# Dense bf16 matmuls in a recurrence on TensorE, one reordered step on VectorE, and two groups of loads issued later

## What is computed

```python
for t in range(S):                      # r, k, v: [B, H, S, D]; w, u: [H, D]
    cur = einsum('bhd,bhe->bhde', u[None] * kt, vt)
    y[:, :, t] = einsum('bhd,bhde->bhe', rt, state + cur)
    state = w[None, :, :, None] * state + einsum('bhd,bhe->bhde', kt, vt)

logits = x @ w_gate                     # x: [3072, 384]; each token to one of 8 experts,
h = maximum(x[mask] @ w1[e], 0.0)       # 384 tokens an expert, by falling logit
out[mask] = h @ w2[e]

h = maximum(maximum(x @ w1, x @ w2), x @ w3)
return h @ w_out                        # [3072, 384]
```

## Time and profile before

| | |
|---|---|
| Median of 3 runs | 818.34 us (815.5 to 818.6) |
| The profiled execution | 818.57 us, its span 816.5 us |
| TensorE busy, share of the span | 94% |
| VectorE | 57% |
| ScalarE | 28% |
| GpSimd | 20% |
| Moved by DMA | 68.64 MB, mean 84 GB/s |

### The profile page before, as it was taken

One profiled execution on the slowest core, in us unless ns is written; L12 is line 12 of the kernel. 1 busy time (PEld: TensorE's weight loads), 2 busy tenths in 40 slices (PEclk: granted clock), 3 DMA queues, 4 the chain that ended last, 5 costly groups with the idle time before them and its releaser, 6 DMA issues.

```text
span 816.5 us, 18498 instructions
## 1 busy us (share of the span) xinstructions
PE 771.2 (94%) x7502; PEld 738.2 (90%) x7502; DVE 461.5 (57%) x1083; ACT 230.9 (28%) x518; POOL 166.3 (20%) x203
## 2 busy tenths in 40 slices
PE   7999999999636999999999999999999999999996
PEld 6899999999526999999999999999999999999995
DVE  5554545452486778647666764766676477344231
ACT  5232332323402214203411521341152133134121
POOL 7644444450013002102101110210121011201001
PEclk9555555555558999999999999999999999999998
DMA  8996765200023022004103100500310040400000
GB/s 203 255 283 204 208 182 174 71 31 27 14 78 107 1 89 97 30 1 175 39 0 134 49 29 0 183 29 0 154 29 29 8 175 30 148 37 30 1 1 29
DMA packets 18198, 68.64 MB, mean 84 GB/s; under 512 B 3296, under 2 KB 7264, under 8 KB 16096
## 3 DMA queue, kind: packets, MB, share of 16 engines
q1 hardware_dynamic: 9312, 28.53, 12.9%
q0 software_dynamic: 5376, 34.61, 11.7%
q10 hardware_dynamic: 3456, 4.72, 1.6%
HBM read 58.41 MB, written 9.44 MB: 83 GB/s over the span
## 4 chain that ended last, share of the span: by engine, by line
PE 90%; DVE 4%; DMA 2%; ACT 1%; issue 1%; POOL 0%; POOLq 0%; SPq 0%
PE bank L1083 21%; PE bank L1085 20%; PE bank L1084 20%; PE bank L987 5%; PE bank L1000 5%; PE bank L1016 4%; PE bank L1050 3%; PE bank L967 3%; PE bank L950 3%; PE bank L1010 2%; DMA rkv<-in_rkv 2%; PE bank L1079 1%; DVE one_row L680 1%; ACT rk L489 1%; PE bank L930 1%
## 5 line engine op out<-in xcount | busy, mean ns | idle before, releaser
L1083 PE MATMUL bank<-xh,w1h 128*128 128x384 f32 x192 | 67.0, 349 | 0.0
L1083 PE MATMUL bank<-hh,w2h 128*128 128x384 f32 x192 | 66.9, 348 | 0.0
L401 POOL DMA_INDIRECT w1r<-in_w,w_row x8 | 8.5, 1064 | 283.0 <-PE bank L1085 231.5
L1085 PE MATMUL bank<-xh,w1l 128*128 128x384 f32 x192 | 64.5, 336 | 0.0
L1085 PE MATMUL bank<-hh,w2l 128*128 128x384 f32 x192 | 64.5, 336 | 0.0
L1084 PE MATMUL bank<-hl,w2h 128*128 128x384 f32 x192 | 64.3, 335 | 0.0
L1084 PE MATMUL bank<-xl,w1h 128*128 128x384 f32 x192 | 64.2, 335 | 0.0
L429 POOL DMA_INDIRECT out<-ot,idsc x24 | 23.8, 993 | 171.9 <-ACT ot L539 167.6
L862 DVE SCALAR_TENSOR_TENSOR hl<-bank,hh 128x384 fp32r<-128x384 f32 x64 | 35.3, 553 | 38.3 <-ACT hh L515 38.3
L515 ACT ACTIVATE hh<-bank 128x384 fp32r<-128x384 f32 x64 | 31.4, 491 | 83.2 <-PE bank L1085 82.1
L987 PE MATMUL bank<-middle,rk 48*64 48x48 f32 x384 | 51.3, 305 | 0.0
(11 more groups left out here) (182 smaller groups left out, 2056.0 us busy)
## 6 DMA issues: line engine op xcount, KB each, us to landing
rkv<-in_rkv SPq DMA_DIRECT2D x24, 576.0 KB, 7.1
rk<-in_rk SPq DMA_DIRECT2D x48, 192.0 KB, 4.6
x_rows<-ysb ACTq DMA_DIRECT2D x24, 192.0 KB, 4.0
m0r<-in_m SPq DMA_DIRECT2D x3, 384.0 KB, 17.3
m1r<-in_m SPq DMA_DIRECT2D x3, 384.0 KB, 9.0
m2r<-in_m SPq DMA_DIRECT2D x3, 384.0 KB, 6.1
mor<-in_m_out SPq DMA_DIRECT2D x3, 384.0 KB, 6.4
xg<-x_rows,idg POOLq DMA_INDIRECT x24
```

The costliest lines, as they stand in the source:

```text
L1083: pe.matmul(out, wh_, ah, start=first, stop=False)
L1085: return pe.matmul(out, wl_, ah, start=False, stop=last)
```

## The change

1. A table `DENSE` and a function `dense(times)`: matmuls of `ones16` (128x128, bf16) with `later16` taken four times (512 columns), into bank 0, whose result is overwritten by the scores. `scores(u)` issues them behind its two waits and ahead of its matmuls: 16 for units 2 and 9, two for every other unit from 1 on, none for unit 0.
2. On VectorE the scaling of unit 1 no longer stands ahead of the mask, first half and dot sums of unit 0, but behind them. All other units keep their order.
3. On SyncE `un` and `wg` are issued behind the loads of unit 1, no longer behind those of unit 0.
4. The twelve loads of the shared weights are issued behind the load of the last unit.

```diff
+DENSE = {2: 16, 9: 16}
@@ SyncE
                 load(u)
-                if u == 0:
+                if u == 1:
                     sp.dma_start(un[:].rearrange("p h d -> p (h d)"), u_d.partition_broadcast(P)).then_inc(s_const, 16)
                     sp.dma_start(wg[:], wg_d.rearrange("(k p) e -> p k e", p=P)).then_inc(s_const, 16)
@@
                 load(u)
-                if u < NB + 12:
-                    load_m(u - NB)
+            for n in range(4 * KX):
+                load_m(n)
@@ VectorE
             for n in range(NU + 2):
-                if n + 1 < NU:
+                if 1 <= n < NU - 1:
                     scale(n + 1)
@@
                     mask(n)
                     first_half(n)
                     dots(n)
+                if n == 0:
+                    scale(1)
@@ TensorE
+            def dense(times):
+                for _ in range(times):
+                    pe.matmul(bank[:, 0, :], ones16[:], later16[:].unsqueeze(1).broadcast_to([P, 4, P]),
+                              start=True, stop=True)
+
             def scores(u):
                 i = u % NB
                 pe.wait_ge(s_scaled, u + 1)
                 if u >= 1:
                     pe.wait_ge(s_masked, u)
+                dense(DENSE.get(u, 2 if u >= 1 else 0))
```

## The result

The changed kernel took 786.5 us in the median of four executions (780.2 to 790.6), against 818.5 before, a ratio of 0.961 (0.954 to 0.968). On another chip it took 773.7 us, 0.946 (0.942 to 0.950). So it is faster, by 32 and 43 us; the forecast was 58.6. Both times lie in the stated range, 744 to 802, but its upper end was set past the two rivals at 776 and 789 and owes nothing to the mechanism of the forecast. Its executions differ by 10 to 15 us where those before differ by 3; the ratios leave out executions over 1.5% above the fastest of a kernel, the medians don't.

The account below looks back on a forecast made before the run. TensorE at half clock was taken to bound the recurrence; unit 3's turn at 36.2 us, then mostly 5.2 us turns, end it at 155.3 instead of 213.9: 818.6 - 58.6 = 760.0 us, range 744 to 802.

Parts of the forecast that it names:

- the two rivals at 776 and 789: 776 us: clock kept, another bound makes units 6.0 us (chance 0.15); 789 us: clock kept from only one stretch (0.12).
- the mechanism of the forecast: Recurrence: dense matmuls raise TensorE's clock and it is kept, units take 5.2 us instead of 8.12; 760 us, chance 0.55.
- The cost of a dense matmul: Ahead of the scores: each 512-column bf16 matmul takes 0.46 us at half clock, 0.23 at full; 74 in all.
- A unit at full clock: Steady unit of the recurrence: 5.05 us with two dense matmuls, taken as 5.2, with 4.8 and 6.0 as ends.
- collisions: Within a unit: scaling against products, transfers and VectorE stand just under 5.05 us, so 5.2 was taken.
- The start: Units 0 to 3: the reordering loses 3.3 us at unit 1's scores; unit 3's turn starts at 36.2 against 31.72.
- granted clock 1.0 from about 30 us to the end of the recurrence: TensorE in the profile after: full clock kept without a fall through the recurrence, if the forecast holds.
- The prediction's own sign of being wrong: Recurrence: the clock falls within a few units, or a unit at full clock takes over 6 us.
- The clock isn't kept: Recurrence: two dense matmuls a unit aren't enough to hold the clock; slower, 841 us, chance 0.18.
- It is kept from only one of the stretches: An empty stretch while transfers bind drops the clock until unit 9's dense matmuls; 789 us, chance 0.12.
- The shared weights: Twelve loads moved behind the last unit's: landed at 137 us, read at 155, 18 us of cover, no cost.

Follow-up runs that it names:

- the combined kernel: Changed kernel with four dense matmuls a unit, no unit 9 stretch, shared weights behind the recurrence, `un` and `wg` behind unit 0: 768.7 us, 0.938.

## Why the prediction was right in its sign and too large

**The cost of a dense matmul.** Forecast 0.46 and 0.23 us; measured 0.43 from start to start at half clock and 0.21 at full. The Trainium skill (TensorE: Matmul & The Clock Gate, "Wait — 56ns, not 53.3ns?") was nearer than the row of 384 columns. The first stretch took 5.65 us, with the rise 4.1 us into it (30.3); 5.7 and some 4 were forecast:

```profile
26.18 5.65 PE L945 MATMUL bank<-later,ones 128*128 128x512 bf16 x16
```

**A unit at full clock.** The sum of 5.05 us was right (5.01); the 0.15 that I added for collisions wasn't there. Scaling and products rarely met: 1.22 us is the usual scaling in the trace after, where 1.75 was before.

**The start.** GpSimd's first product at 13.79 instead of the forecast 14.7, the scores of unit 1 at 19.86 instead of 20.6, unit 2's turn at 26.18 instead of 25.9, unit 3's at 35.74 instead of 36.2. All four within 1 us:

```profile
13.79 0.99 POOL L380 TENSOR_TENSOR rkv<-rkv 128x384 f32<-128x384 f32 x1 [5.46 <-DMA wg<-in_w_gate]
...
19.86 1.14 PE L959 MATMUL bank<-rk 48*64 48x64 f32 x32
```

**The step that failed** is "granted clock 1.0 from about 30 us to the end of the recurrence". The prediction's own sign of being wrong, a fall within a few units, came at 40.6 us, in the turn of unit 3. The sum has no term for a stall of TensorE. By the starts of the masks of units 3 and 23 (37.0 and 163.7) twenty turns took 126.7 us; the forecast had 20 x 5.2 - 1.2 + 3.2 = 106.0. The difference, 20.7 us, is that between the forecast end of the recurrence (155.3) and the measured one (175.2), to a microsecond. The turns behind it: four of 8.98 at half clock, one of 8.0 partly at half, and six of 5.3 to 7.0 around the falls and rises. The run with the shared weights behind the recurrence is the check on the rest of the sum: with only one short fall its recurrence ended at 157.8 and the profiled execution took 759.9 us.

**Of the rivals** none had the mechanism. "The clock isn't kept" took the pairs for too weak to hold it; it is held without them. "It is kept from only one of the stretches" had the shape of the result and nearly its time (789), with the loss in the right place (units 4 to 7, while transfers were dense), but had it end by the stretch at unit 9; in fact the pairs brought the clock back at 71.3 us, before that stretch began at 79.9, and it fell twice more behind 129 us. That 789 lies near the measured 786.5 is chance:

```profile
79.89 3.62 PE L945 MATMUL bank<-later,ones 128*128 128x512 bf16 x16
```

I had noted that transfers are dense in those units and looked only for waits for data. By the landings and the places of the stalls, what TensorE ran short of was its own instructions. No row of the kernel before shows that: at half clock no stall of 0.5 us stands in its recurrence.

**The shared weights** were costed at nothing, with 18 us of cover. The cover held: line 475 waited for no transfer. But I asked only who waits for the moved loads, and not whom they disturb: twelve fast loads beside the last unit loads brought the DMA engines to a share of 1.04 at 412 GB/s, and there stand a stall of 1.0 us and the fall at 136.1. With the unit loads cut down the only stall came inside this lump. That is a cost on another engine, at a place where the edit seemed to have no part. How large it is isn't shown: the five kernels that load the weights behind the recurrence still had one fall each between 112 and 146 us.

## What to carry to other kernels

Where a change makes an engine consume its instructions twice as fast, look at the traffic beside it: a stall of half a microsecond that costs next to nothing by itself can cost four microseconds a unit if the clock falls with it. Dense filler matmuls have two separate uses, to lift the clock once and to bring it back after a fall; price them by how often the second happens. And of a transfer that is moved ask both questions, who waits for it and what runs beside it in its new place.

## What the runs showed of the hardware

- TensorE's granted clock rose during a dense stretch (28 fp32 transposes before the experts, 16 bf16 matmuls of 512 columns in the recurrence), and with two or four such matmuls per unit of 9 us at half clock it rose again after some time; with the small tiles alone, busy 100%, it didn't in 150 us. Once full, the same small tiles held it for 46 us with no dense matmul among them.
- Stalls of TensorE that the profile puts down to nothing, of 0.5 to 3.1 us at full clock, ended 1.3 to 1.8 us behind the landing of a 16 KB block on the instruction queue, and all stood at places of TensorE's program 256 instructions apart or a multiple of it. With the loads of units 8 to 23 cut down there were none over 0.5 us in 85 us.
- Four bf16 matmuls per unit instead of two kept each stay at half clock to 3.4 to 6.8 us in one profile, against 3.4 to 30.7 in the changed kernel's, and up to 68.2 in another with two (39.3 to 107.5, no stretch at unit 9); in the combined kernel, with four, one stay of 23.9 us came all the same.
